# A two-scale attention and feed-forward kernel: TensorE's attention burst between the up and the down group of a first-layer step

## The chip, the cores and the metric

The kernel runs on 1 core of one Trainium2 chip. The metric is the time of one execution on the device, in microseconds (us). The engines are TensorE (PE; PEld is its weight load), VectorE (DVE), ScalarE (ACT), GpSimd (POOL) and SyncE (SP, which issues the DMAs here).

## The reference

An attention at two scales makes 2304 tokens of 512 values, and two feed-forward layers follow.

```python
def _attn_ref(q, k, v):                       # (4, 8, 576, 64) each
    q_d = q.reshape(B, H, Sd, factor, D).mean(axis=3)      # factor 4; k_d, v_d alike
    out_d = sm_attn(q_d, k_d, v_d)            # softmax attention over 144 tokens
    out_up = np.repeat(out_d, factor, axis=2)
    mask = np.abs(pos[:, None] - pos[None, :]) < factor
    scores = np.where(mask, scale * np.matmul(q, k.transpose(0, 1, 3, 2)), -1000000000.0)
    ...                                       # softmax
    return (out_up + np.matmul(attn, v)).astype(np.float32)

x = attn_out.transpose(0, 2, 1, 3).reshape(B * S, H * D)   # (2304, 512)
h = x @ w_in;   g = np.maximum(0.01 * h, h);  x = g @ w_out      # 512 -> 2048 -> 512
h = x @ w_in2;  g = h - np.tanh(h);           y = g @ w_out2
```

## The kernel before

Attention works on pairs of heads; there are 16. A pair's work is cut into 17 small steps (0 to 16). On TensorE, steps 0 to 3 transpose q and k (L370), step 4 makes the local scores (L377), step 6 the coarse scores (L444), steps 11 to 14 transpose the probabilities pl and pd (L396, L401), and steps 15 and 16 multiply them by the values (L409, L417). The steps between belong to the other engines: step 3 sums q, steps 4 and 5 take the scores out of PSUM, sum k and subtract the maximum (VectorE, L809, L816, L817, L826), steps 7 and 8 are the exponentials (ScalarE, L603, L607) with VectorE's maxima and sums (L832, L837, L841), and steps 9 and 10 normalize pl and pd on GpSimd (L981, L986). ScalarE copies each transposed block out of PSUM (L591 to L624). Two PSUM banks carry all of it, and semaphores (bank_full, bank_free, norm_l and so on) say when a bank is written and when it is free.

Four pairs are done ahead of the first layer, with the first steps of a fifth. The other 12 are spread over the first layer. That layer has 8 tiles of 288 tokens, and each tile 16 chunks f of its 2048 hidden columns. On TensorE a step f of a tile has up to three parts, in this order: the up group of chunk f (`hidden1`, 12 matmuls of 288 columns: each fp32 product is made of hi*hi, lo*hi and hi*lo, L479 to L481, for four parts of the contraction), the down group of chunk f-2 (`down1`, again 12, L508 to L510, into the accumulator acc), and a burst of attention (`later`). `later` gives a pair's work to eight steps by the table GROUPS, shifted by two: the bursts of f = 0 to 7 hold steps (4, 5), (6, 7, 8), (9, 10), (11, 12), (13, 14), (15, 16), and then (0, 1), (2, 3) of the next pair; f = 8 to 15 do the same for that pair. Steps (9, 10) have nothing on TensorE. Tiles 0 to 5 have such bursts, tile 5 only up to f = 13; tiles 6 and 7 have none. The down groups lag two steps, so f = 0 and 1 have none and a tile has two more down groups behind f = 15; the up group of the next tile's first chunk stands ahead of the last of them.

Behind an up group the other engines turn h into g, hi and lo: ScalarE copies 0.01 h (L676), VectorE takes the maximum (L877), ScalarE rounds to g_hi (L660), VectorE subtracts to g_lo (L864). In the same step each of them has, in program order behind that, its own share of the pair's steps. Half of the weights (chunks 0 to 7) is kept in two parts, hi and lo; the weights of chunks 8 to 15 are split anew for each tile: ScalarE rounds in_hi and out_hi (L644, L648), GpSimd subtracts in_lo and out_lo (L997, L1002). GpSimd's order in a step is in_lo of chunk f+2, its attention step, out_lo of chunk f. In tile 0 the kept weights of chunks 2 to 7 are split as well (ScalarE L634, GpSimd L992, w_lo_a), each two steps ahead. ScalarE's out_hi of chunk f (from chunk 10 on) waits until down group f-2 is done, since it shares its buffer.

SyncE loads q and k of the next pair once step 3 of a pair is through TensorE, and v once step 16 is.

The second layer has 6 tiles of 384 tokens and no attention; it begins behind the last down group of the first (L555 to L557 are its down matmuls).

Of the kernel before, what the change touches and what calls it, by code (L numbers as in the profile page):

```python
# [52 lines left out]
def wait_from(eng, semaphore, value):  # L53

    if isinstance(value, int) and value <= 0:
        return
    eng.wait_ge(semaphore, value)


def two_scale_attention_and_feed_forward(nc, q, k, v, w_in1, w_out1, w_in2, w_out2, out):  # L60
# [36 lines left out]
    with ExitStack() as ctx:  # L97
# [124 lines left out]
        def uses0(i, n):  # L222


            return 7 * i + n

        def uses1(i, n):

            return 6 * i + n
# [14 lines left out]
        def later(f, tile, last):  # L244

            if f < last:
                pair, group = divmod(f + GROUP_HEAD, len(GROUPS))
                for step in GROUPS[group]:
                    yield step, A, 2 * tile + 2 + pair
# [116 lines left out]
        def _(pe):  # L366
            def turn_tokens(s, src, g, bank):

                for f in range(FACTOR):
                    last = pe.transpose(s.banks[:, bank, f * LP:(f + 1) * LP], src[:, g * FACTOR + f, :, :],  # L370
                                        ident[0:LP, 0:LP])
                last.then_inc(s.bank_full[bank], 1)
# [8 lines left out]
            def scores(s):  # L381

                for n in range(NBA - 1):
                    score(s, 0, n, P if n == 0 else QB)
                    score(s, 1, n)
                score(s, 0, NBA - 1)
                for n in range(NBA, NB):
                    last = score(s, 0, n)
                    if n == NB - 1:
                        last.then_inc(s.bank_full[1], 1)  # L390
                    score(s, 1, n - 1)
                score(s, 1, NB - 1).then_inc(s.bank_full[0], 1)

            def turn_l(s, bank, n0, n1):
                for n in range(n0, n1):
                    last = pe.transpose(s.banks[0:WIN, bank, (n - n0) * P:(n - n0 + 1) * P], s.pl[:, n, :], ident[:, :])  # L396
                return last

            def turn_d(s, bank, g, at):
                for t in range(QT):  # L400
                    last = pe.transpose(s.banks[0:HALF, bank, at + t * QP:at + (t + 1) * QP],  # L401
                                        s.pd[:, t, g * HALF:(g + 1) * HALF], ident[0:QP, 0:QP])
                return last

            def values_l(s, bank, n0, n1):
                for n in range(n0, n1):
                    for h in range(2):
                        probs = s.pT[:, slot_of(h, n), h * QB:(h + 1) * QB]
                        last = pe.matmul(s.banks[h * D:(h + 1) * D, bank, (n - n0) * QB:(n - n0 + 1) * QB],  # L409
                                         s.vw[:, n, h, :], probs, start=True, stop=True)  # L410
                return last

            def values_d(s, bank):
                probs = s.pdT.rearrange("p g (n h m) -> p g n h m", n=NB, h=2)
                for h in range(2):
                    for g in range(2):
                        last = pe.matmul(s.banks[h * D:(h + 1) * D, bank, QB:QB + SD_], s.vd[:, g, h, :],  # L417
                                         probs[:, g, :, h, :], start=(g == 0), stop=(g == 1))
                return last

            def attention(step, s, i):
                if step == 0:
                    pe.wait_ge(s.q_loaded, 32 * i + 32)
                    wait_from(pe, s.bank_free[1], uses1(i, 0))
                    turn_tokens(s, s.qn, 0, 1)
                elif step == 1:
                    wait_from(pe, s.bank_free[0], uses0(i, 0))
                    turn_tokens(s, s.qn, 1, 0)
                elif step == 2:
                    pe.wait_ge(s.k_loaded, 32 * i + 32)  # L430
                    pe.wait_ge(s.bank_free[1], uses1(i, 1))
                    turn_tokens(s, s.kn, 0, 1)
                elif step == 3:
                    pe.wait_ge(s.bank_free[0], uses0(i, 1))
                    turn_tokens(s, s.kn, 1, 0)
                elif step == 4:
                    pe.wait_ge(s.bank_free[0], uses0(i, 2))
                    pe.wait_ge(s.bank_free[1], uses1(i, 2))
                    scores(s)
                elif step == 6:  # L440
                    pe.wait_ge(s.means_done, 2 * i + 2)
                    pe.wait_ge(s.bank_free[0], uses0(i, 3))
                    for t in range(QT):
                        last = pe.matmul(s.banks[0:QP, 0, t * SD_:(t + 1) * SD_],  # L444
                                         s.qd_diag[:, 3 * t:3 * t + 3, :, :].rearrange("p n h m -> p (n h m)"),
                                         s.kdT[:, :], start=True, stop=True)
                    last.then_inc(s.bank_full[0], 1)
                elif step == 11:
                    pe.wait_ge(s.norm_l, i + 1)
                    pe.wait_ge(s.bank_free[1], uses1(i, 3))  # L450
                    turn_l(s, 1, 0, 4).then_inc(s.bank_full[1], 1)
                elif step == 12:
                    pe.wait_ge(s.bank_free[0], uses0(i, 4))
                    turn_l(s, 0, 4, 8).then_inc(s.bank_full[0], 1)
                elif step == 13:
                    pe.wait_ge(s.bank_free[1], uses1(i, 4))
                    pe.wait_ge(s.norm_d, i + 1)
                    turn_l(s, 1, 8, 9)
                    turn_d(s, 1, 0, P).then_inc(s.bank_full[1], 1)
                elif step == 14:  # L460
                    pe.wait_ge(s.bank_free[0], uses0(i, 5))
                    turn_d(s, 0, 1, 0).then_inc(s.bank_full[0], 1)
                elif step == 15:
                    pe.wait_ge(s.v_loaded, 128 * i + 128)
                    pe.wait_ge(s.vd_done, i + 1)
                    pe.wait_ge(s.bank_free[1], uses1(i, 5))
                    values_l(s, 1, 8, 9)
                    pe.wait_ge(s.bank_free[0], uses0(i, 6))
                    values_d(s, 1).then_inc(s.bank_full[1], 1)
                elif step == 16:  # L470
                    values_l(s, 0, 0, 8).then_inc(s.bank_full[0], 1)

            def hidden(bank, hi, lo, x_hi, x_lo, width, x_wait):

                for c in range(CD):
                    if x_wait is not None:
                        pe.wait_ge(x_lo_done, x_wait + c + 1)
                    whi, wlo = hi[:, c * P:(c + 1) * P], lo[:, c * P:(c + 1) * P]
                    pe.matmul(bank, whi, x_hi[:, c, 0:width], start=(c == 0), stop=False)  # L479
                    pe.matmul(bank, whi, x_lo[:, c, 0:width], start=False, stop=False)  # L480
                    last = pe.matmul(bank, wlo, x_hi[:, c, 0:width], start=False, stop=(c == CD - 1))  # L481
                last.then_inc(h_done, 1)

            def hidden1(tile, f):
                n = CF * tile + f
                if f < KEPT:
                    hi, lo = w_hi_a[:, f, 0:DM], w_lo_a[:, f, 0:DM]
                    pe.wait_ge(kept_lo_done, f + 1)
                else:
                    hi, lo = in_hi[:, f % 2, :], in_lo[:, f % 2, :]  # L490
                    pe.wait_ge(in_lo_done, WHOLE * tile + f - KEPT + 1)
                wait_from(pe, g_lo_done, n - 1)
                hidden(ph1[:, f % 2, 0:T1], hi, lo, x1_hi, x1_lo, T1, CD * tile if f == 0 else None)
# [21 lines left out]
            def layer1(tile, last, begun=True, ahead=True):  # L515
                for f in range(CF + LAG1):
                    if f < CF and not (begun and f == 0):
                        hidden1(tile, f)
                    if ahead and f == CF + LAG1 - 1:
                        hidden1(tile + 1, 0)  # L520
                    if f >= LAG1:
                        down1(tile, f - LAG1)
                    for step, s, i in later(f, tile, last):
                        attention(step, s, i)

            def hidden2(tile, f):
                if f < KEPT:
# [47 lines left out]
            with pe.Fori(1, MIXED - 1) as tile:  # L575
                layer1(tile, CF)
# [517 lines left out]
```

## Time and profile before

| | |
|---|---|
| median of 3 runs | 982.59 us (976.28 to 983.01) |
| the profiled execution | 982.79 us |
| its span, first to last instruction | 981.0 us |
| mean granted TensorE clock | 0.981 |
| instructions | 19759 |
| first layer with attention | about 66 to 460 us |

In the profile's rows a time is in us from the start of the span, PE, PEld, DVE, ACT, POOL and SP are the engines, and L508 is line 508 of the kernel. `out<-in` are the program's names with buffer numbers left out. In a row of the timeline the first number is the start, the second how long; where rows of one line follow closely they are drawn together, with x and their number. A bracket gives the idle time of the engine just before and what ended it; without a bracket there was none to speak of. Matmuls are pipelined and their ends modelled, so the start of the next group is a better end than the one shown.

### The profile page before, as it was taken

Reading aid. Unit: us, or ns where it says so; the run is one execution under the profiler, and the core shown is the slowest. Engines: PE = TensorE matmul, PEld = TensorE weight load, DVE = VectorE, ACT = ScalarE, POOL = GpSimd, SP = SyncE. Lnnn points to the kernel's source line nnn. Section 1 sums busy time; section 2 is a strip of 40 time slices with the busy share of each in tenths; the row PEclk is TensorE's granted clock in tenths of the full one; section 3 lists DMA queues with packets and bytes.
Section 4 is the critical chain, followed back from the end, with each engine's and each line's share of the span. In section 5 each row is a group of like instructions: output and inputs, shape, how many; then the busy total and the mean of one; then the engine's idle time right before and its main releaser. Section 6 shows DMA issues by size and latency. Waiting matters only on the chain.

```text
span 981.0 us, 19759 instructions
## 1 busy us (share of the span) xinstructions
PE 951.6 (97%) x6960; PEld 893.9 (91%) x6960; DVE 552.4 (56%) x1066; ACT 560.1 (57%) x1355; POOL 406.8 (41%) x341
## 2 busy tenths in 40 slices
PE   6788999999999999999999999999999999999998
PEld 5678999999999999999999999899899899898996
DVE  5654554454455544544324667776676666766764
ACT  3445545554635446446354767765676665766754
POOL 4435632723626417336171837623233233233232
PEclk9769999999999999999999999999999999999999
DMA  7652421112111211212001303100000000000000
GB/s 168 158 158 59 123 51 37 27 38 49 29 25 44 49 25 24 50 27 65 1 2 32 109 24 87 32 34 1 3 30 1 32 0 0 32 0 0 33 1 33
DMA packets 87797, 41.48 MB, mean 42 GB/s; under 512 B 60352, under 2 KB 81344, under 8 KB 87744
## 3 DMA queue, kind: packets, MB, share of 16 engines
q1 hardware_dynamic: 87744, 40.78, 15.6%
q8 instruction: 33, 0.54, 0.2%
q14 instruction: 20, 0.16, 0.1%
HBM read 36.04 MB, written 4.72 MB: 42 GB/s over the span
## 4 chain that ended last, share of the span: by engine, by line
PE 83%; POOL 6%; ACT 4%; DVE 3%; issue 3%; DMA 1%; ACTq 0%; POOLq 0%; DVEq 0%
PE ph L479 13%; PE ph L481 12%; PE ph L480 12%; PE acc L555 6%; PE acc L556 6%; PE acc L557 6%; PE acc L508 6%; PE acc L509 6%; PE acc L510 6%; PE banks L377 3%; PE banks L409 2%; PE banks L396 2%; PE banks L370 2%; POOL in_lo L997 1%; POOL pl L981 1%
## 5 line engine op out<-in xcount | busy, mean ns | idle before, releaser
L1018 POOL TENSOR_TENSOR g_lo<-scratch,g_hi 128x384 fp32r<-128x384 f32 x96 | 125.9, 1311 | 257.1 <-ACT g_hi L660 257.1
L877 DVE TENSOR_TENSOR ph<-g,ph 128x288 f32<-128x288 f32 x128 | 58.9, 460 | 166.8 <-ACT g L676 166.5
L479 PE MATMUL ph<-x_hi,w_hi_a 128*128 128x288 f32 (+1 forms) x448 | 144.4, 322 | 2.1 <-DVE x_lo L859 1.9
L997 POOL TENSOR_TENSOR in_lo<-w_whole,in_hi 128x512 fp32r<-128x512 f32 x64 | 84.5, 1320 | 144.2 <-ACT in_hi L644 143.6
L481 PE MATMUL ph<-x_hi,w_lo_a 128*128 128x288 f32 (+1 forms) x448 | 141.0, 315 | 0.0
L480 PE MATMUL ph<-x_lo,w_hi_a 128*128 128x288 f32 (+1 forms) x448 | 140.9, 315 | 0.0
L676 ACT ACTIVATE g<-ph 128x288 f32<-128x288 f32 x128 | 52.5, 410 | 138.1 <-PE ph L481 138.0
L1002 POOL TENSOR_TENSOR out_lo<-w_whole,out_hi 128x512 fp32r<-128x512 f32 x64 | 85.9, 1343 | 72.5 <-ACT out_hi L648 72.3
L911 DVE SCALAR_TENSOR_TENSOR scratch<-scratch,ph 128x384 f32<-128x384 f32 x96 | 53.2, 554 | 109.5 <-ACT scratch L722 105.0
L721 ACT ACTIVATE scratch<-ph 128x384 f32<-128x384 f32 x96 | 46.8, 487 | 108.4 <-PE ph L481 106.9
L864 DVE TENSOR_TENSOR g_lo<-ph,g_hi 128x288 fp32r<-128x288 f32 x128 | 58.6, 458 | 59.1 <-ACT g_hi L660 59.1
L479 PEld LDWEIGHTS ph<-x_hi,w_hi_a 128*128 128x128 f32 x448 | 85.1, 190 | 5.0 <-issue 2.7
L480 PEld LDWEIGHTS ph<-x_lo,w_hi_a 128*128 128x128 f32 x448 | 85.1, 190 | 1.4
L481 PEld LDWEIGHTS ph<-x_hi,w_lo_a 128*128 128x128 f32 x448 | 85.2, 190 | 0.0
L660 ACT ACTIVATE g_hi<-ph 128x288 fp32r<-128x288 f32 x128 | 52.7, 411 | 47.4 <-DVE ph L877 46.8
L479 PE MATMUL ph<-x_hi,in_hi 128*128 128x288 f32 x256 | 79.1, 309 | 0.0
L508 PE MATMUL acc<-g_hi,out_hi 128*128 128x288 f32 x256 | 76.9, 300 | 0.7 <-POOL out_lo L1002 0.5
L509 PE MATMUL acc<-g_lo,w_hi_a 128*128 128x288 f32 x256 | 76.1, 297 | 0.0
L508 PE MATMUL acc<-g_hi,w_hi_a 128*128 128x288 f32 x256 | 75.9, 296 | 0.0
L510 PE MATMUL acc<-g_hi,out_lo 128*128 128x288 f32 x256 | 75.9, 296 | 0.0
L510 PE MATMUL acc<-g_hi,w_lo_a 128*128 128x288 f32 x256 | 75.8, 296 | 0.0
L509 PE MATMUL acc<-g_lo,out_hi 128*128 128x288 f32 x256 | 75.8, 296 | 0.0
(162 smaller groups left out, 2688.5 us busy)
## 6 DMA issues: line engine op xcount, KB each, us to landing
out_dram<-o_stage SPq DMA_DIRECT2D x18, 256.0 KB, 2.1
w_whole<-in_moe_w_in_dram SPq DMA_DIRECT2D x16, 256.0 KB, 3.6
w_whole<-in_moe_w_out_dram SPq DMA_DIRECT2D x16, 256.0 KB, 4.3
qn<-in_q_dram SPq DMA_DIRECT2D x28, 144.0 KB
kn<-in_k_dram SPq DMA_DIRECT2D x28, 144.0 KB
v4n<-in_v_dram SPq DMA_DIRECT2D x28, 144.0 KB
vw<-in_v_dram SPq DMA_DIRECT2D x28, 122.5 KB
scratch<-in_moe_w_in_dram SPq DMA_DIRECT2D x8, 256.0 KB, 2.7
```

The lines of the kernel that those rows point to most:

```text
L479: pe.matmul(bank, whi, x_hi[:, c, 0:width], start=(c == 0), stop=False)
L480: pe.matmul(bank, whi, x_lo[:, c, 0:width], start=False, stop=False)
L481: last = pe.matmul(bank, wlo, x_hi[:, c, 0:width], start=False, stop=(c == CD - 1))
L508: pe.matmul(acc[:, c, 0:T1], whi, g1_hi[:, f % 3, :], start=(f == 0), stop=False)
L509: pe.matmul(acc[:, c, 0:T1], whi, g1_lo[:, f % 3, :], start=False, stop=False)
L510: last = pe.matmul(acc[:, c, 0:T1], wlo, g1_hi[:, f % 3, :], start=False, stop=(f == CF - 1))
L555: pe.matmul(acc[:, j, 0:DM], hi, whi, start=(f == 0), stop=False)
L556: pe.matmul(acc[:, j, 0:DM], hi, wlo, start=False, stop=False)
L877: dve.tensor_tensor(ph1[:, f % 2, 0:T1], g1[:, f % 2, :], ph1[:, f % 2, 0:T1], ALU.max)\
L997: pool.tensor_tensor(in_lo[:, f % 2, :], w_whole[:, f - KEPT, 0:DM], in_hi[:, f % 2, :].bitcast(F32), ALU.subtract).then_inc(in_lo_done, 1)
L1002: pool.tensor_tensor(out_lo[:, f % 2, :], w_whole[:, f - KEPT, DM:CW], out_hi[:, f % 2, :].bitcast(F32), ALU.subtract).then_inc(out_lo_don ...
L1018: pool.tensor_tensor(g2_lo[:, f % 3, :], g2[:, f % 2, :], g2_hi[:, f % 3, :].bitcast(F32), ALU.subtract).then_inc(g_lo_done, 1)
```

## The change

In the loop that writes TensorE's program for a first-layer tile, the two lines of the attention burst move from behind the down group to behind the up group. In a step that has all three parts the order becomes up, burst, down. It applies to all tiles of the first layer. Nothing else is changed: no other engine's program, no semaphore and no count.

```diff
                 for f in range(CF + LAG1):
                     if f < CF and not (begun and f == 0):
                         hidden1(tile, f)
+                    for step, s, i in later(f, tile, last):
+                        attention(step, s, i)
                     if ahead and f == CF + LAG1 - 1:
                         hidden1(tile + 1, 0)
                     if f >= LAG1:
                         down1(tile, f - LAG1)
-                    for step, s, i in later(f, tile, last):
-                        attention(step, s, i)
```

The instructions of VectorE, ScalarE, GpSimd and SyncE keep their order. On TensorE the order before, at f = 11 of tile 0, from the last matmul of up group 11 to the first of up group 12 (out_hi and out_lo are the split down weights, pl the probabilities, norm_l the semaphore that GpSimd's L981 raises):

```order
L481 MATMUL ph<-x_hi,in_lo 128x288
L508 MATMUL acc<-g_hi,out_hi 128x288 [waits g_lo_done,out_lo_done]
L509 MATMUL acc<-g_lo,out_hi 128x288
L510 MATMUL acc<-g_hi,out_lo 128x288
...
L396 MATMUL banks<-ident,pl 70x128 [waits bank_free1_a,norm_l_a]
L396 MATMUL banks<-ident,pl 70x128 x3
L396 MATMUL banks<-ident,pl 70x128 [waits bank_free0_a]
L396 MATMUL banks<-ident,pl 70x128 x3
L479 MATMUL ph<-x_hi,in_hi 128x288 [waits g_lo_done,in_lo_done]
```

And at the same place now:

```order
L481 MATMUL ph<-x_hi,in_lo 128x288
L396 MATMUL banks<-ident,pl 70x128 [waits bank_free1_a,norm_l_a]
L396 MATMUL banks<-ident,pl 70x128 x3
L396 MATMUL banks<-ident,pl 70x128 [waits bank_free0_a]
L396 MATMUL banks<-ident,pl 70x128 x3
L508 MATMUL acc<-g_hi,out_hi 128x288 [waits g_lo_done,out_lo_done]
L509 MATMUL acc<-g_lo,out_hi 128x288
L510 MATMUL acc<-g_hi,out_lo 128x288
...
L479 MATMUL ph<-x_hi,in_hi 128x288 [waits g_lo_done,in_lo_done]
```

The eight transposes with their wait for norm_l stood behind the twelve matmuls of down group 9 and stand ahead of them now; up group 12 comes behind both either way.

The first half of a tile, at f = 3 of tile 0, as it is now (w_hi_a and w_lo_a are the kept weights):

```order
L481 MATMUL ph<-x_hi,w_lo_a 128x288
L396 MATMUL banks<-ident,pl 70x128 [waits bank_free1_a,norm_l_a]
L396 MATMUL banks<-ident,pl 70x128 x3
L396 MATMUL banks<-ident,pl 70x128 [waits bank_free0_a]
L396 MATMUL banks<-ident,pl 70x128 x3
L508 MATMUL acc<-g_hi,w_hi_a 128x288 [waits g_lo_done]
...
L479 MATMUL ph<-x_hi,w_hi_a 128x288 [waits g_lo_done,kept_lo_done]
```

Here it is down group 1 that the transposes have passed. The bursts of f = 0 and f = 1 have no down group in their step and stand where they stood.

## Rows read from the trace of the kernel before

**Rows 1.** The page: busy us, share, instructions; chain that ended last.
```profile
PE 951.6 (97%) x6960; PEld 893.9 (91%) x6960; DVE 552.4 (56%) x1066; ACT 560.1 (57%) x1355; POOL 406.8 (41%) x341
...
PE 83%; POOL 6%; ACT 4%; DVE 3%; issue 3%; DMA 1%; ACTq 0%; POOLq 0%; DVEq 0%
```

**Rows 2.** Stretches: from:to, length, busy us (count) by engine, clock, DMA share, GB/s.
```profile
300.00:350.00 50.00, 49.60 (x462) 48.22 (x460) 27.76 (x58) 27.26 (x72) 27.06 (x25) 1.00 0.15 36
```

**Rows 3.** Waits of TensorE, 90 to 600 us: total us, times, longest.
```profile
PE banks L396 <- POOL pl L981: 2.0, 6, 0.4
PE acc L508 <- POOL out_lo L1002: 0.5, 1, 0.5
```

**Rows 4.** Timeline, TensorE, tile 3, f = 11: start, us, operation [idle before, releaser].
```profile
312.18 0.30 PE L479 MATMUL ph<-x_hi,in_hi 128*128 128x288 f32 x1
...
313.78 0.30 PE L508 MATMUL acc<-g_hi,out_hi 128*128 128x288 f32 x1
...
315.90 1.06 PE L396 MATMUL banks<-ident,pl 128*70 128x128 f32 x8 [0.36 <-POOL pl L981]
```

**Rows 5.** Timeline, the same tile, f = 8 to 11, the chain to L981.
```profile
303.25 0.46 DVE L864 TENSOR_TENSOR g_lo<-ph,g_hi 128x288 fp32r<-128x288 f32 x1 [0.48 <-ACT g_hi L660]
...
303.36 1.69 PE L377 MATMUL banks<-kT,qT 64*128 64x70 f32 x36
...
305.08 0.52 DVE L816 TENSOR_TENSOR pl<-banks,band 128x350 f32<-128x350 f32 x1 [1.38 <-PE banks L377]
...
306.86 0.41 ACT L676 ACTIVATE g<-ph 128x288 f32<-128x288 f32 x1 [3.12 <-PE ph L481]
...
307.50 0.88 DVE L826 TENSOR_TENSOR pl<-pl,mxl 128x630 f32<-128x630 f32 x1
...
308.30 0.45 DVE L877 TENSOR_TENSOR ph<-g,ph 128x288 f32<-128x288 f32 x1
...
309.23 0.46 DVE L864 TENSOR_TENSOR g_lo<-ph,g_hi 128x288 fp32r<-128x288 f32 x1 [0.48 <-ACT g_hi L660]
...
311.31 0.62 ACT L648 ACTIVATE out_hi<-w_whole 128x512 fp32r<-128x512 f32 x1
...
312.02 1.29 POOL L1002 TENSOR_TENSOR out_lo<-w_whole,out_hi 128x512 fp32r<-128x512 f32 x1 [2.50 <-ACT out_hi L648]
...
313.27 1.29 POOL L997 TENSOR_TENSOR in_lo<-w_whole,in_hi 128x512 fp32r<-128x512 f32 x1
...
314.52 1.25 POOL L981 TENSOR_TENSOR pl<-pl,rs 128x630 f32<-128x630 f32 x1
```

**Rows 6.** Timeline, ScalarE, f = 11 of the same tile.
```profile
315.22 0.41 ACT L660 ACTIVATE g_hi<-ph 128x288 fp32r<-128x288 f32 x1 [0.31 <-DVE ph L877]
...
316.56 0.59 ACT L612 ACTIVATE pT<-banks 70x512 f32<-70x512 f32 x1 [0.93 <-PE banks L396]
...
317.05 0.58 ACT L616 ACTIVATE pT<-banks 70x512 f32<-70x512 f32 x1
```

**Rows 7.** Timeline, tile 4, f = 3.
```profile
346.46 1.24 POOL L981 TENSOR_TENSOR pl<-pl,rs 128x630 f32<-128x630 f32 x1 [7.64 <-DVE rs L841]
...
347.24 0.29 PE L508 MATMUL acc<-g_hi,w_hi_a 128*128 128x288 f32 x1
```

**Rows 8.** Timeline, tile 0, f = 3.
```profile
78.89 0.29 PE L508 MATMUL acc<-g_hi,w_hi_a 128*128 128x288 f32 x1
...
79.49 2.40 POOL L992 TENSOR_TENSOR w_lo_a<-w_whole,w_hi_a 128x1024 fp32r<-128x1024 f32 x1 [4.74 <-ACT w_hi_a L634]
...
83.14 1.07 PE L396 MATMUL banks<-ident,pl 128*70 128x128 f32 x8 [2.50 <-POOL pl L981]
```

**Rows 9.** Stretches in and before tile 0, columns as in rows 2.
```profile
84.46:87.87 3.41, 3.41 (x17) 3.41 (x16) 0.46 (x1) 1.97 (x4) 3.41 (x2) 0.51 0.00 0
...
16.00:17.00 1.00, 0.04 (x1) 0.04 (x1) 0.99 (x3) 1.00 (x3) 0.80 (x2) 1.00 0.20 43
```

**Rows 10.** Timeline, GpSimd, f = 11 of the tile before that of rows 5.
```profile
248.47 1.25 POOL L981 TENSOR_TENSOR pl<-pl,rs 128x630 f32<-128x630 f32 x1
```

## The prediction

> **What bounds the kernel now.** I read the busy table first: TensorE's matmul row is busy for 97% of the span, the other engines for 41 to 57%, and the chain that ended last runs through TensorE for 83% [rows 1]. Then the table by stretches: in a stretch in the middle of the first layer TensorE is busy for 49.60 of 50 us at the full clock [rows 2]. Then its waits there: over the whole first layer behind tile 0's first steps it waits 2.0 us, six times, for GpSimd's normalization L981, and 0.5 us once for something else [rows 3]. So the time is the length of TensorE's queue plus those waits. The change adds no instruction and takes none away; it can only make waits shorter or longer.
>
> A group of twelve matmuls takes 313.78 - 312.18 = 1.60 us [rows 4]. I call it G. A step of the first layer is an up group, a down group and perhaps a burst. Steps count f = 0 to 15; a pair's bursts lie at f = 0, 1, 3, 4, 5, 6, 7 of eight steps, and again from f = 8 on.
>
> **What moves.** Where a step has all three parts the burst comes one G sooner after its up group, and the down group one burst later; the next up group starts when it did. That holds for f = 3 to 9 and 11 to 15: twelve bursts in tiles 0 to 4, ten in tile 5, 70 in all. At f = 0 and 1 there is no down group, at 2 and 10 no burst. Nothing is won on TensorE itself. What can be won is what others do with the earlier results; what can be lost is that a burst's own inputs are not there one G sooner.
>
> **The burst of steps 11 and 12, second half (f = 11), 6 times.** It transposes pl, so it needs L981. Before, down group 9 began at 313.78, the burst was wanted at 313.78 + 1.60 = 315.38 and began at 315.90, a wait of 0.52 (the row says 0.36, against a modelled end) [rows 4]. Now it is wanted at 313.78. When is L981 ready? I follow its chain back [rows 5].
> - At f = 8 the scores began at 303.36, so now at 301.76, and VectorE's L816, which followed them by 1.72 (305.08), could start at 303.48. But VectorE is in g_lo L864 from 303.25 for 0.46, so L816 starts at 303.71, 1.37 sooner. L826, the last of that row of VectorE work, moves from 307.50 to 306.13 and ends at 307.01.
> - VectorE's L877 of f = 9 stood behind L826 at 308.30. Its input, ScalarE's L676, is ready at 306.86 + 0.41 = 307.27, and that binds now: L877 at 307.30, 1.00 sooner. g_lo L864 behind it was at 309.23; with a little lost where ScalarE finishes in_hi, I take 308.27, which is 0.96 sooner. L607, out_hi L648 (311.31), out_lo L1002 (312.02), in_lo L997 (313.27) and L981 (314.52) stood back to back behind it, and move by 0.96. The burst can start at 315.90 - 0.96 = 314.94.
> - The new wait is 314.94 - 313.78 = 1.16 instead of 0.52. Loss 0.64, six times: 3.8 us. The bounds are 0 (the chain moves by the full 1.60, nothing stopping it at 303.71 and 307.27) and 1.60 (it doesn't move at all).
>
> **The same burst, first half (f = 3), tiles 1 to 5.** The bursts at f = 0 and 1 don't move, so neither does its chain: L981 starts at 346.46, the moment VectorE's L841 releases it, after 7.64 us of idle GpSimd. Down group 1 began at 347.24; that is when the burst is wanted now [rows 7]. From the start of L981 to the start of the burst it is 315.90 - 314.52 = 1.38, so it comes at 347.84. Before, it was wanted one G later and waited for nothing. Loss 0.60, five times: 3.0 us. (Perfetto Trace Analysis in the Trainium skill, section "GPSIMD Engine Instruction", says that GpSimd's spans are unreliable and are better timed start to start. By that, the row's neighbours give 314.52 - 313.27 = 1.25 for such an operation, and with no delay to TensorE the loss would be 0.47 each, 0.65 us less in all; the trace shows the release at 1.38, which I take.)
>
> **Tile 0, f = 3.** L981 starts at 79.49 + 2.40 = 81.89, behind w_lo_a L992, which GpSimd begins at 79.49 and which takes 2.40. Nothing moved stands in that chain. The burst began at 83.14; down group 1 had begun at 78.89, so it was wanted at 80.49, and is wanted now at 78.89 [rows 8]. The wait goes from 2.65 to 4.25: loss 1.60. Behind the old wait the clock fell: 84.46 to 87.87 ran at 0.51, the 1.2 GHz level, which costs 3.41 x 0.49 = 1.7 us [rows 9]. The longer wait may bring the fall forward into it, so that the work from 83.14 to 84.46, 1.3 us, also runs at half speed: +0.7. Nothing, and a second stretch as long as the first (+1.7), are the bounds. I take 0.7.
>
> **The other bursts cost nothing**, and what hides them is a G. At f = 9 the products need the sums of k (between L816 and L826, so done before 306.13) and start after the up group, whose end set ScalarE off at 306.86. At f = 12 the burst needs ScalarE's copies of the burst before; they were at 316.56 and 317.05 + 0.58, and are now behind g_hi of f = 11 (315.22), so they end by 317.2, and the burst is wanted at 314.94 + 1.06 + 1.60 + 1.60 = 319.20 (1.06 for the burst's row) [rows 4, 6]. If such a cover failed, each would cost up to a G. The down groups, now later, release out_hi's buffers later: behind a burst as long as the scores' (1.72) ScalarE's out_hi L648 comes up to that much later, but the next down group needs its product only two steps on. SP's loads wait for step 3 and step 16 of TensorE, which come sooner; no queue of SP is moved past.
>
> **Sum:** 3.8 + 3.0 + 1.6 + 0.7 = 9.1 us. The profiled execution took 982.8 (span 981.0 and 1.8 around it), so 991.9; against the median of 982.6 that is 991.7, slower by 0.9%. A measurement of this kernel tells about 1% from no change.
>
> **Rivals.**
> 1. *Earlier results pay back more.* The bursts at f = 4, 8, 9 and 12 hand VectorE and ScalarE work one G sooner, in steps where those engines queued behind it (L877 at 308.30 behind L826). If L981 comes fully 1.60 sooner at f = 11 and TensorE's other small waits (the 0.5 us) vanish, the second halves give back what they cost: only 3.0 + 1.6 is left, 987.2; were the first halves hidden too, 984.2. Were the six old waits to go away it would be 982.6 - 6 x 0.52 - 0.5 = 979. For it speaks VectorE's early start; against it the POOL queue, back to back from 312.02 to 314.52, and a first half in which nothing moves. 0.18.
> 2. *The clock falls at each new wait, and it is clearly slower.* One wait of 2.50 us dropped the clock for 3.41 us [rows 8, 9]. If the six waits of 1.16 us do it too, each costs another 1.7: 991.7 + 10 = 1002. The 0.52 us waits did not do it; nor did the second from 16 to 17 us, in which TensorE was busy for 0.04 us [rows 9]. It decides if a wait of 1.16 us is enough. 0.10.
> 3. *TensorE isn't held in order.* If the down group went past the waiting transposes, nothing would be lost, and the result 982.6. Against it: at 83.14 up group 4, whose inputs were there, had waited behind the burst. (PSUM — Partial Sum Buffer in the Trainium skill, "Engine vs sequencer instructions", says that only weight loads go ahead and matmuls run in program order; by that this rival is dead, and the trace agrees with its 2.50 us idle.) 0.02.
> 4. *A down group or a copy becomes late* as a second new wait, up to 0.5 us in each of 12 pairs: 997. 0.04.
>
> **How the numbers follow.** The sum's own case has 0.66. Its bounds: second halves 0 to 1.60 each (0 to 9.6 us), first halves 0.47 to 0.66, tile 0 from 1.6 to 3.3; most likely 988 to 996. The 1% line is at 992.4, 0.7 above the sum, so I split this case 0.38 below and 0.28 above it. Slower by over 1%: 0.28 + 0.10 + 0.04 = 0.42. Faster by over 1% would need 973; I leave 0.03 of rival 1 for it. Within 1%: 0.55. The range 985.5 to 998 leaves out rival 2 and half of rivals 1 and 3.
>
> **What would show it.** TensorE's waits for L981 behind tile 0's start: eleven instead of six, six near 1.0 us and five near 0.45 by the row's own idle, and 4.1 us at f = 3 of tile 0. L981 of f = 11 starts 0.2 us before up group 11 ends (313.56 against 313.78), where it started 0.7 behind it. L877 of f = 9 some 1.0 us sooner after its up group. A period of a tile that grows from 66.05 (two rows of L981 a tile apart, 314.52 and 248.47) to 67.3 [rows 5, 10]. Granted clock of 1.00 from 90 us to the end. I am wrong if the tile's period stays, or if a second wait stands beside L981's.

## The result and the profile after

| | kernel before | changed kernel |
|---|---|---|
| median | 980.91 us (976.28 to 983.01, 4 runs) | 998.63 us (995.79 to 998.83, 4 runs) |
| span of the profiled execution | 981.0 us | 996.8 us |
| mean granted TensorE clock | 0.981 | 0.980 |

The ratio is 1.0167, with a 95% interval of 1.0137 to 1.0196: slower by 1.7%, 17.7 us between the medians and 15.8 between the spans. The prediction had the direction, 991.7 us, and a range up to 998.0, which the median passes by 0.6. The other runs of the kernel before, made beside the experiments, had medians of 981 to 982.

The busy row and the chain of the changed kernel hardly tell the difference: the same work is spread over a longer span, and GpSimd's L981 has 2% of the chain where it had 1% [rows 1]:

```profile
PE 953.7 (96%) x6960; PEld 893.7 (90%) x6960; DVE 558.9 (56%) x1066; ACT 558.3 (56%) x1355; POOL 407.0 (41%) x341
...
PE 82%; POOL 6%; DVE 5%; ACT 4%; issue 3%; ACTq 0%; POOLq 0%; DVEq 0%
PE ph L479 11%; PE ph L481 11%; PE ph L480 11%; PE acc L555 7%; PE acc L556 6%; PE acc L557 6%; PE acc L508 6%; PE acc L509 6%; PE acc L510 6%; PE banks L377 2%; PE banks L409 2%; PE banks L396 2%; POOL pl L981 2%; POOL in_lo L997 1%; PE banks L370 1%
```

The table of TensorE's waits does, from 90 to 620 us (total, times, longest) [rows 3]:

```profile
PE banks L396 <- POOL pl L981: 13.5, 11, 1.9
PE acc L508 <- POOL out_lo L1002: 0.5, 1, 0.5
```

Eleven waits for L981, as forecast, 13.5 us instead of 2.0, and no new wait for anything else: the one of 0.5 us for out_lo was there before [rows 3], and one of 0.4 us in the second layer (for g_lo) is in both kernels. But the longest is 1.9, not 1.0. The timeline of the changed kernel shows it in tile 3, f = 8 to 11, with the chain behind it. The lines answer to [rows 4, 5], and stand some 8.6 us later on the clock of the trace:

```profile
310.34 1.69 PE L377 MATMUL banks<-kT,qT 64*128 64x70 f32 x36
...
311.83 0.46 DVE L864 TENSOR_TENSOR g_lo<-ph,g_hi 128x288 fp32r<-128x288 f32 x1 [0.48 <-ACT g_hi L660]
...
312.21 0.51 DVE L816 TENSOR_TENSOR pl<-banks,band 128x350 f32<-128x350 f32 x1
...
314.32 0.73 POOL L974 TENSOR_TENSOR vd<-vd,v4n 72x256 f32<-72x256 f32 x1
...
314.62 2.34 DVE L826 TENSOR_TENSOR pl<-pl,mxl 128x630 f32<-128x630 f32 x1
...
315.01 1.28 POOL L1002 TENSOR_TENSOR out_lo<-w_whole,out_hi 128x512 fp32r<-128x512 f32 x1
...
315.46 0.41 ACT L676 ACTIVATE g<-ph 128x288 f32<-128x288 f32 x1 [3.14 <-PE ph L481]
...
316.88 0.45 DVE L877 TENSOR_TENSOR ph<-g,ph 128x288 f32<-128x288 f32 x1
...
320.78 0.30 PE L479 MATMUL ph<-x_hi,in_hi 128*128 128x288 f32 x1
...
323.10 1.24 POOL L981 TENSOR_TENSOR pl<-pl,rs 128x630 f32<-128x630 f32 x1
...
324.47 1.06 PE L396 MATMUL banks<-ident,pl 128*70 128x128 f32 x8 [1.94 <-POOL pl L981]
```

L826, VectorE's subtraction of the maximum, began 0.84 us ahead of ScalarE's L676 of f = 9 (314.62 against 315.46), where it had begun 0.64 behind it (307.50 against 306.86): 1.48 sooner. But it took 2.34 us instead of 0.88 and ended at the same place after L676 as before, 1.50 us behind its start (1.52 before). Everything behind it stands where it stood: L877 is 1.42 behind L676 (1.44 before), and L981 is 2.32 behind the start of up group 11 (323.10 - 320.78; before 314.52 - 312.18 = 2.34). So TensorE waits 324.47 - 320.78 - 1.60 = 2.09 us instead of 0.52.

In the first half (f = 3), tile 3 [rows 7]:

```profile
287.58 0.29 PE L479 MATMUL ph<-x_hi,w_hi_a 128*128 128x288 f32 x1
...
288.38 1.25 POOL L981 TENSOR_TENSOR pl<-pl,rs 128x630 f32<-128x630 f32 x1 [7.67 <-DVE rs L841]
...
289.76 1.06 PE L396 MATMUL banks<-ident,pl 128*70 128x128 f32 x8 [0.42 <-POOL pl L981]
```

The burst was wanted at 287.58 + 1.60 = 289.18 and came at 289.76, a wait of 0.58 (0.60 forecast). In tile 0, first the timeline, then the table by stretches [rows 8, 9]:

```profile
76.60 0.37 PE L479 MATMUL ph<-x_hi,w_hi_a 128*128 128x288 f32 x1
...
82.83 1.49 PE L396 MATMUL banks<-ident,pl 128*70 128x128 f32 x6 [4.40 <-POOL pl L981]
```
```profile
82.83:87.87 5.04, 5.04 (x24) 4.83 (x25) 0.26 (x1) 2.14 (x3) 4.63 (x3) 0.54 0.00 0
81.00:82.83 1.83, 0.00 (x1) 0.01 (x1) 1.32 (x4) 1.04 (x3) 1.83 (x3) 0.50 0.06 14
```

From the end of up group 3 (76.60 + 1.60 = 78.20) TensorE waits 4.63 us instead of 2.65, and the granted clock was already at 0.50, the 1.2 GHz level, within the wait. So 5.04 us of work ran at 0.54, which costs 2.3 us where it had cost 1.7.

| part | forecast | measured |
|---|---|---|
| f = 11, six times | 0.64 each, 3.8 | 2.09 - 0.52 = 1.57 each, 9.4 |
| f = 3, five times | 0.60 each, 3.0 | 0.58 each, 2.9 |
| tile 0, the wait | 1.6 | 2.0 |
| tile 0, the clock | 0.7 | 0.6 |
| sum | 9.1 | 14.9 of 15.8 us |

The f = 11 and f = 3 rows are those of tile 3, taken for all; the other tiles' waits agree with them within 0.1 us by the rows. The remaining 0.9 us is no wait of TensorE in the first layer. TensorE reached the end of up group 3 of tile 0 0.7 us sooner, and the second layer (from the first L555 to the end) took 402.1 us instead of 400.9. What is left after that, 0.4 us, was not traced.

### The profile page after: what moved, and what is told of

It is laid out like the page before. It is cut to its first block, busy times and chain, and to the rows that moved or that the text cites. A ratio compares the mean times of both kernels' runs of the same rounds, so it can differ in the third digit from the quotient of the medians.

```text
span 996.8 us, 19759 instructions
## 1 busy us (share of the span) xinstructions
PE 953.7 (96%) x6960; PEld 893.7 (90%) x6960; DVE 558.9 (56%) x1066; ACT 558.3 (56%) x1355; POOL 407.0 (41%) x341
## 4 chain that ended last, share of the span: by engine, by line
PE 82%; POOL 6%; DVE 5%; ACT 4%; issue 3%; ACTq 0%; POOLq 0%; DVEq 0%
PE ph L479 11%; PE ph L481 11%; PE ph L480 11%; PE acc L555 7%; PE acc L556 6%; PE acc L557 6%; PE acc L508 6%; PE acc L509 6%; PE acc L510 6%; PE banks L377 2%; PE banks L409 2%; PE banks L396 2%; POOL pl L981 2%; POOL in_lo L997 1%; PE banks L370 1%
## 5 line engine op out<-in xcount | busy, mean ns | idle before, releaser
L877 DVE TENSOR_TENSOR ph<-g,ph 128x288 f32<-128x288 f32 x128 | 59.0, 461 | 196.5 <-ACT g L676 196.1
L676 ACT ACTIVATE g<-ph 128x288 f32<-128x288 f32 x128 | 52.6, 411 | 164.3 <-PE ph L481 164.3
L479 PE MATMUL ph<-x_hi,w_hi_a 128*128 128x288 f32 (+1 forms) x448 | 141.6, 316 | 2.1 <-DVE x_lo L859 1.9
L1002 POOL TENSOR_TENSOR out_lo<-w_whole,out_hi 128x512 fp32r<-128x512 f32 x64 | 85.7, 1340 | 75.1 <-ACT out_hi L648 74.7
L508 PE MATMUL acc<-g_hi,w_hi_a 128*128 128x288 f32 x256 | 80.0, 313 | 0.0
L508 PE MATMUL acc<-g_hi,out_hi 128*128 128x288 f32 x256 | 78.9, 308 | 0.9 <-POOL out_lo L1002 0.5
L480 PE MATMUL ph<-x_lo,in_hi 128*128 128x288 f32 x256 | 75.6, 295 | 0.0
```

The lines of the kernel that those rows point to most:

```text
L508: pe.matmul(acc[:, c, 0:T1], whi, g1_hi[:, f % 3, :], start=(f == 0), stop=False)
L1002: pool.tensor_tensor(out_lo[:, f % 2, :], w_whole[:, f - KEPT, DM:CW], out_hi[:, f % 2, :].bitcast(F32), ALU.subtract).then_inc(out_lo_don ...
```

## The experiments

Each is a variant of one of the two kernels. "Period" is the time from the L981 of f = 11 of tile 1 to that of tile 2; it leaves out the start of the program, where the clock is at its lower level for a time that differs from run to run and makes some microseconds of difference. It is 66.1 us in the kernel before (248.47 - 182.38) and 68.3 in the changed one (254.78 - 186.47).

### Which of the moved bursts costs

Theory A: only those of steps 11 and 12 (f = 3 and f = 11), by waiting for L981. Rival B: any moved burst costs a little.

```diff
+                    if f % 8 != 3:        # "all_but_11"; in "only_11" the condition is f % 8 == 3
+                        for step, s, i in later(f, tile, last):
+                            attention(step, s, i)
                     if ahead and f == CF + LAG1 - 1:
                         hidden1(tile + 1, 0)
                     if f >= LAG1:
                         down1(tile, f - LAG1)
+                    if not (f % 8 != 3):
+                        for step, s, i in later(f, tile, last):
+                            attention(step, s, i)
```

> All bursts of the change are moved but those of steps 11 and 12 (f = 3 and f = 11), which stand behind the down group again; 58 of 70 moved bursts stay moved. Theory A (the whole loss is TensorE waiting for L981 at f = 3 and 11, and the others cost nothing): the waits for L981 behind tile 0's first steps are six of 0.3 to 0.5 us again, the wait at f = 3 of tile 0 2.5 us, the period of a tile 66.0 to 66.2 us, and the time 980 to 983, within 0.3% of the kernel before. Rival B (the loss comes with any moved burst: refilling behind it, down groups later, some 16 us over 70 bursts, 0.23 each): 58 x 0.23 = 13 us, 994. In both, L826 of f = 8 takes 2.3 us, as in the changed kernel.

> Only the bursts of steps 11 and 12 (f = 3 and f = 11, 12 in all) are moved; every other burst stands where it stood before. Theory A: L826 and the chain behind it stand where they stood before, so L981 of f = 11 comes as late as before: TensorE waits 2.1 us from the end of up group 11 instead of 0.5, 1.6 x 6 = 9.6; f = 3 0.6 x 5 = 3.0; tile 0 2.3 to 2.7: 15 to 15.5 us above the kernel before, 996. L826 takes 0.88 us. Rival B (any moved burst costs 0.23): 12 x 0.23 = 3 us, 984. If the other bursts' earlier results did help L981, this kernel is slower than the changed one; by theory A by no more than 0.6 us (0.1 a tile).

With all but these moved: 979.77 us against 982.01 of the kernel before, ratio 0.9979 (0.9959 to 1.0), period 66.1. With only these moved: 996.40, ratio 1.014 (1.0109 to 1.0172), period 68.3. Their waits, first of all_but_11, then of only_11 (lines of these files are 4 higher, so L985 is L981 and L830 is L826):

```profile
PE banks L396 <- POOL pl L985: 1.9, 6, 0.4
```
```profile
PE banks L396 <- POOL pl L985: 13.5, 11, 1.9
```

Twelve bursts carry the whole loss and the other 58 none; rival B is out. One detail missed: in all_but_11 the wait at f = 3 of tile 0 was 1.0 us by the row, not 2.5. There the granted clock was 0.65 from 70 to 74 us, so TensorE came later; that this is why was not tested. VectorE's subtraction at f = 8 took, in all_but_11 and then in only_11:

```profile
236.13 2.35 DVE L830 TENSOR_TENSOR pl<-pl,mxl 128x630 f32<-128x630 f32 x1
```
```profile
246.07 0.87 DVE L830 TENSOR_TENSOR pl<-pl,mxl 128x630 f32<-128x630 f32 x1
```

So its 2.35 us come with the scores' burst of f = 8 being sooner, and not with the late L981.

### Why L826 took 2.34 us

Theory C: GpSimd, which does its sums of v (L974) and out_lo (L1002) at that time. Rival D: TensorE or ScalarE. The sums are moved one step ahead, to where GpSimd was idle, in the changed kernel (vd_early) and in the kernel before (vd_early_before):

```diff
                     for step, s, i in later(f, tile, last):        # GpSimd
-                        attention(step, s, i)
+                        if step == 3:
+                            attention(5, s, i)
+                        elif step != 5 or (isinstance(tile, int) and tile == 0 and f == 0):
+                            attention(step, s, i)
```

> The changed kernel, with GpSimd's sums of v (L974, 2.3 us a pair) made one step sooner: with step 3 (f = 7 and 15) instead of step 5 (f = 8 and 0), where GpSimd was idle. GpSimd is then idle while VectorE does L826 at f = 8. Theory C (L826 takes 2.34 us instead of 0.88 because GpSimd works at the same time, and this ate the lead of 1 us): L826 is back at 0.8 to 0.9 us, L877 of f = 9 starts 1.0 us sooner after its up group, L981 of f = 11 0.9 to 1.0 sooner, TensorE's wait there 1.0 to 1.1 by the row instead of 1.94: 6 x 0.9 = 5.4 us below the changed kernel, about 993. The wait at f = 3 stays 0.42. Rival D (L826 is slow because it now runs beside TensorE's matmuls or ScalarE, not because of GpSimd): L826 stays at 2.3 and the time at 998.

> The kernel before with the same move of GpSimd's sums of v to step 3, bursts behind the down group. Theory C: L826 of f = 8 (307.50 in the kernel before) took 0.88 with GpSimd's out_lo beside it for 0.2 us, so it has nothing to win: 0.8 to 0.9, and in_lo L997 of that step, 1.65 us then, is what may be shorter. L981 of f = 11 no more than 0.1 sooner, time 980 to 983. If GpSimd's own row were what makes L981 late, its waits for L981 would vanish here and the time fall by 3 us to 978.

vd_early: 990.44 us, ratio 1.0079 (1.0046 to 1.0112), 8.2 below the changed kernel's median where 5.4 were expected. The profiled executions are 5.9 apart (spans of 990.9 and 996.8), and the period, free of the start, is 67.3, 1.0 less: six times 1.0, near what the theory asked for. The rest of the 8.2 is not in the tiles. In the trace of vd_early:

```profile
243.65 0.81 DVE L826 TENSOR_TENSOR pl<-pl,mxl 128x630 f32<-128x630 f32 x1
...
252.55 1.06 PE L396 MATMUL banks<-ident,pl 128*70 128x128 f32 x8 [0.97 <-POOL pl L981]
```

L826 took 0.81 us with GpSimd idle beside it, and the wait is 0.97 by the row instead of 1.94. This is the kernel that the prediction had in mind. It forecast a period of 67.3 and a wait of 1.16; counted the same way, from the end of up group 11, the wait is 252.55 - 249.82 - 1.60 = 1.13 (up group 11 began at 249.82). Rival D is out, since the edit touches only GpSimd's order. vd_early_before: 982.59, ratio 1.0001 (0.9983 to 1.0019), six waits of 0.3: there L826 had next to nothing to win.

### What of GpSimd holds it up

In the changed kernel L826 began during the third sum and ended 0.67 us behind out_lo: it seemed to wait for two instructions. First the order of the two was swapped (out_first), then a wait put between them (vd_gap), so that out_lo doesn't follow on the sum at once.

```diff
+                    if f == KEPT:                     # out_first, GpSimd
+                        split_out(tile, f)
                     for step, s, i in later(f, tile, last):
                         attention(step, s, i)
-                    if KEPT <= f:
+                    if KEPT < f:
                         split_out(tile, f)
```
```diff
                     ins.then_inc(s.vd_done, 1)
+                    pool.wait_ge(s.vd_done, i + 1)    # vd_gap
```

> The changed kernel with GpSimd's order at f = 8 swapped: out_lo of chunk 8 (L1002) ahead of the sums of v (L974) instead of behind them. By the changed kernel's rows GpSimd then does in_lo 311.45 to 312.7, out_lo to 314.0, sums to 316.3, and is idle until in_lo at 316.5; L826 starts at 314.6. Theory C (VectorE's L826 is held up while GpSimd works, whatever it works on): L826 ends when GpSimd stops, 1.7 to 1.9 us instead of 2.35; the chain behind it comes 0.4 to 0.6 sooner, TensorE's wait at f = 11 falls from 1.94 to 1.4 or 1.5 by the row, and the time by 3 us to 995. Rival E (only the 512-column out_lo holds it up, not the 72-partition sums): L826 0.9, wait 1.0, time 993. Rival D (not GpSimd at all): 2.35, 998.

> The changed kernel with one more wait on GpSimd: behind the third sum of v (L974) it waits until that sum is done before it begins out_lo of chunk 8 (L1002). No work moves. In the changed kernel L1002 began 0.04 us before the row of the third sum ended (315.01 against 315.05), VectorE's L826 had begun at 314.62 during that sum and ended at 316.96, 0.67 behind the end of L1002. Where the swapped order ran, the sums are apart by such waits (0.08 us) and L826 took 0.82. Theory F (VectorE is held up by the GpSimd instruction that runs, and by the next one too if that follows without a gap; a gap of under 0.1 us is enough to let it in): L826 ends about 0.8 us behind the third sum, 1.2 to 1.3 us long, L1002 is what becomes late (some 0.8 us), L981 of f = 11 comes 1.0 sooner, TensorE's wait there is 1.0 by the row instead of 1.94, time 998.6 - 5.7 = 993. Rival E (only out_lo's operands collide with L826, and GpSimd's next instruction always goes first): 2.35 us and 998.

out_first: 993.15 us, ratio 1.0116 (1.0057 to 1.0174), period 67.3, waits of 1.0. Theory C in its plain form, by which L826 ends only when GpSimd stops, had asked for 1.4 to 1.5 and missed; L826 did not need GpSimd to stop:

```profile
243.83 0.72 POOL L974 TENSOR_TENSOR vd<-v4n 72x256 f32<-72x256 f32 x1
...
244.50 0.82 DVE L826 TENSOR_TENSOR pl<-pl,mxl 128x630 f32<-128x630 f32 x1
...
244.63 2.08 POOL L974 TENSOR_TENSOR vd<-vd,v4n 72x256 f32<-72x256 f32 x2
```

L826 came at the end of a sum, got in before the next one, and now the two later sums, 1.54 us together in the changed kernel, took 2.08. By that result alone rival E (out_lo only) fitted as well. vd_gap separates them: 993.02 us, ratio 1.0118 (1.0083 to 1.0154), period 67.3, waits of 1.0.

```profile
311.47 0.73 POOL L974 TENSOR_TENSOR vd<-vd,v4n 72x256 f32<-72x256 f32 x1
...
311.76 1.11 DVE L826 TENSOR_TENSOR pl<-pl,mxl 128x630 f32<-128x630 f32 x1
...
312.28 1.74 POOL L1003 TENSOR_TENSOR out_lo<-w_whole,out_hi 128x512 fp32r<-128x512 f32 x1
```

(L1003 is out_lo here.) L826 again begins 0.3 us after the third sum began. Now it is held to the sum's end (312.20) and ends 0.67 behind that; out_lo, which begins 0.08 behind the sum, takes 1.74 instead of 1.28. No work was moved, only a gap of 0.08 us made, and the period is 1.0 us shorter. So in these runs L826 and GpSimd's sums and splits exclude each other, the one that runs goes on to its end, and at the end of GpSimd's instruction L826 gets in only if GpSimd's next one isn't already following. The kernel before agrees. There L826 began at 307.50, within out_lo, and the next instruction came 0.17 us behind that:

```profile
304.91 1.54 POOL L974 TENSOR_TENSOR vd<-vd,v4n 72x256 f32<-72x256 f32 x2
...
306.41 1.29 POOL L1002 TENSOR_TENSOR out_lo<-w_whole,out_hi 128x512 fp32r<-128x512 f32 x1
...
307.87 1.65 POOL L997 TENSOR_TENSOR in_lo<-w_whole,in_hi 128x512 fp32r<-128x512 f32 x1 [0.17 <-ACT in_hi L644]
```

L826 ended at 308.38, again 0.68 behind the end of out_lo, and it was in_lo that took 1.65 us instead of 1.29. (SBUF — State Buffer in the Trainium skill, "Who interferes with whom", says that a VectorE instruction with two SBUF inputs and a GpSimd instruction that reads SBUF contend for a shared port, and the second to issue blocks until the first is done. The trace agrees with the exclusion, either way round; that L826 also waited for a second instruction without a gap, 2.34 against 1.11, is not in that rule.)

### L981 sooner in GpSimd's order

If L981 alone is what the moved burst lacks, an earlier L981 must make the change harmless. GpSimd does step 9 with the group (6, 7, 8), ahead of out_lo, where it was idle until VectorE's L841.

```diff
                     for step, s, i in later(f, tile, last):        # GpSimd
-                        attention(step, s, i)
+                        if step == 8:
+                            attention(9, s, i)
+                        elif step != 9:
+                            attention(step, s, i)
```

> The changed kernel with GpSimd's L981 (the normalization of pl) one step sooner in GpSimd's order: behind in_lo of f = 9 (and f = 1), ahead of out_lo, where GpSimd is idle until VectorE's L841 is done. In the changed kernel L841 ended at 319.96, and L981 began at 323.10 behind out_lo and in_lo. Theory A: what is late for the moved burst is L981 alone. L981 then starts some 3.0 us sooner at f = 11, the burst has no wait there, 6 x 2.1 = 12.6 us; at f = 3 it stays at 0.42 by the row, as L841 sets it; in tile 0 it no longer stands behind w_lo_a, the wait falls from 4.4 to about 1.2, and the clock doesn't fall: 4 to 5 us. Time 998.6 - 17 = 981, the kernel before within 0.3%. If another input of the moved burst is late as well, a new wait shows at f = 11 and the time stays above 986.

> The kernel before, bursts behind the down group, with the same earlier L981. Theory A: TensorE's six waits of 0.52 us vanish, but out_lo of chunk 9 now stands behind L981 and ends at 314.0, 0.2 behind the moment down group 9 wants it (313.78), so 0.3 of each comes back; tile 0's wait of 2.5 us and the fall of the clock behind it (1.7) go. 982 - 1 - 4.3 = 976 to 977. The first layer's other steps don't change: a tile's period 65.8 to 66.0.

> The earlier L981 with the bursts moved ahead of the down group everywhere but at f = 3, where the first half's L981 can't be sooner. Theory A: no wait for L981 anywhere behind tile 0's first steps, and down group 9, a burst later, has its out_lo: a tile's period 65.6 to 65.8, of the kernel before 66.05. Tile 0 as in before_pl. 982 - 3.1 - 4.3 = 974.5, plus up to 0.2 a tile for the dearer start of a down group behind a burst: 974.5 to 976. The rival, that the moved bursts are worth nothing once L981 is early: equal to before_pl, 976.5.

| | bursts | median, us | ratio to the kernel before | period, us | waits for L981 behind 90 us |
|---|---|---|---|---|---|
| after_pl | as changed | 980.44 | 0.9996 (0.9972 to 1.002) | 66.20 | 5, 2.0 us |
| before_pl | as before | 979.84 | 0.9993 (0.9969 to 1.0017) | 65.83 | none |
| but_3_pl | moved but at f = 3 | 976.13 | 0.9952 (0.9921 to 0.9984) | 65.55 | none |

after_pl as against the changed kernel: 18 us less, all from GpSimd's order. L826 there still takes 2.35 us and it costs nothing, since L981 now waits for VectorE and comes sooner than the burst needs it:

```profile
236.87 2.35 DVE L826 TENSOR_TENSOR pl<-pl,mxl 128x630 f32<-128x630 f32 x1
...
242.28 1.25 POOL L981 TENSOR_TENSOR pl<-pl,rs 128x630 f32<-128x630 f32 x1 [1.91 <-DVE rs L841]
```

What is left of the change's loss are the five waits at f = 3, 0.4 each by the rows. before_pl was expected at 976 to 977 and was 979.84, not clear of the kernel before. Its period is as expected, and in its profiled execution the stretch from the burst of tile 0 to the first L555 is 2.2 us shorter than in the kernel before. But that burst came only 0.4 us sooner (82.71 against 83.14; the granted clock was 0.50 from 66 to 73 us), and the second layer took 402.8 us instead of 400.9; why was not tested.

but_3_pl is the version that beats both kernels, by 0.5% and 2.3%: each burst stands ahead of the down group where its inputs are there, and L981 is done as soon as its own input is. Is the moved burst worth anything in it, beside the earlier L981? The runs of before_pl (974.81 to 982.26) and of but_3_pl (971.36 to 980.88) overlap, but the period is 0.28 us shorter. Most of that is at f = 11. In before_pl up group 11 and the step to down group 9 take 246.12 - 244.29 = 1.83 us instead of 1.60, as out_lo, now behind L981, is done only at 244.76 + 1.30 = 246.06. In but_3_pl the burst stands ahead of that down group, and the up group takes 1.60.

## Why the prediction came out as it did

- **TensorE bounds the kernel, and the change can only alter its waits**: right. Twelve moved bursts with their wait for L981 carry the loss, and the 58 others cost nothing (all_but_11, period 66.1).
- **f = 3, tiles 1 to 5**: right, 0.58 for 0.60. Its chain was not moved, so nothing had to be assumed about it.
- **Tile 0**: the wait grew by 2.0 instead of 1.6, as TensorE was there 0.7 us sooner than in the trace of before and L981 only 0.3 (81.54 against 81.85). The clock fell earlier, into the wait, as forecast, and cost 0.6 for 0.7, but that agreement is luck. Work that takes 1.3 us at full speed costs another 1.3 at half, not 0.7; and the cost stayed at 0.6 because the low stretch ended near 87.5, about where it had ended in the kernel before (87.9), which nothing in the prediction gave.
- **f = 11, the failed step**: "L826 ... moves from 307.50 to 306.13 and ends at 307.01". The start was about right (even a little sooner, since L816 began 0.38 behind the start of g_lo and not 0.46). The end was not: the step kept L826's duration of 0.88 while it moved it in time, and didn't look at what GpSimd did at the new place. The trace of before had it: at 306.13 GpSimd was in the last of its sums (to 306.45), with out_lo following at 306.41. With the old duration the step holds as worked out: in vd_early, out_first and vd_gap, where L826 takes 0.8 to 1.1 us, TensorE's period is the forecast 67.3. The term of the sum was 0.64 and measured 1.57, which is at the bound given for "it doesn't move at all" (1.60).
- The bounds were right but the range was not drawn from them: the sum with that bound is 6 x 1.60 + 3.0 + 1.6 + 0.7 = 14.9, so 997.5, and with a second long stretch at the lower clock (1.7 for 0.7) 998.5.
- **Rivals.** The pay-back did not come. The clock did not fall at the six waits, though they were 1.9 us long by the rows: no profile of this case shows it low between 90 us and the last 20 us. TensorE was held in order. No second wait appeared. (Two of their sums were loose: 987.2 leaves out tile 0's 0.7, and twelve times 0.5 on top of 991.7 is 997.7, not 997. Neither bears on the result.)
- "L981 of f = 11 starts 0.2 us before up group 11 ends" was the sign to look for, and it started 0.7 behind it, as before. That one row told that the lead was lost ahead of GpSimd's queue.

## What to carry to other kernels

Before an engine's work is moved ahead of another's, find the slowest input that it waits for and ask when that is ready: a burst that was covered by 1.6 us of other work pays for all the time by which its input comes behind its new place. When a chain moves in time, its durations are not fixed: an instruction like L826, on VectorE with two SBUF inputs, is to be laid against GpSimd's rows at the new place. And the cheapest cure may stand on another engine: GpSimd, which was idle there, did the needed product one slot sooner and made the loss vanish, and a wait that opened a gap of 0.08 us on it gave back 1 us a tile.

## What the runs showed of the hardware

- A VectorE subtraction of 128x630 fp32 with both inputs in SBUF (the second one 128x9, repeated) took 0.81 us with GpSimd idle (vd_early), and 2.34 when it started 0.3 us into a GpSimd sum that was followed at once by another GpSimd instruction (the changed kernel); with 0.08 us between the two it took 1.11 (vd_gap). Where it got in first, GpSimd's instruction paid: 1.74 us for 1.28.
- With TensorE idle for 1.9 us (by the rows) in each of six places of the changed kernel, amid otherwise dense matmuls, the granted clock stayed at 1.00, the 2.4 GHz level; with 4.4 us idle in tile 0 it was at 0.50, the 1.2 GHz level, before the wait was over.
- Executions of one kernel differ by several microseconds (976.28 to 983.01 for the kernel before), and the profiles differ in how long the clock is low in the first 73 us. Differences of a few microseconds are better read from the period of a tile, which from tile 1 on repeats within 0.1 us in the kernel before (66.09, 66.05, 66.05) and in the changed one (68.31, 68.32, 68.31).
